# One visit to the attention per tile, with its three parts of TensorE work in a row, in a fused attention and two-MLP kernel

## The reference

```python
for t in range(S):
    kt, vt, rt = k[:, :, t], v[:, :, t], r[:, :, t]
    cur = einsum('bhd,bhe->bhde', u * kt, vt)
    y[:, :, t] = einsum('bhd,bhde->bhe', rt, state + cur)
    state = w * state + einsum('bhd,bhe->bhde', kt, vt)
x = y as (B*S, H*D)
h = x @ w_in1;  x = relu(h)**2 @ w_out1
h = x @ w_in2;  x = (h - tanh(h)) @ w_out2
```

## Time and profile before

| | |
|---|---|
| median of 3 runs | 920.28 us (920.14 to 921.25) |
| the profiled execution | 922.49 us |
| its span in the profile | 920.7 us |
| TensorE matmuls | 896.6 us busy (97% of the span) |
| VectorE / ScalarE / GpSimd | 591.2 / 453.1 / 477.1 us busy |
| TensorE's share of the chain that ended last | 82% |

### The profile page before, as it was taken

One profiled execution on the slowest core, in us unless ns is written; L12 is line 12 of the kernel. 1 busy time (PEld: TensorE's weight loads), 2 busy tenths in 40 slices (PEclk: granted clock), 3 DMA queues, 4 the chain that ended last, 5 costly groups with the idle time before them and its releaser, 6 DMA issues.

```text
span 920.7 us, 13868 instructions
## 1 busy us (share of the span) xinstructions
PE 896.6 (97%) x5340; PEld 736.9 (80%) x5340; DVE 591.2 (64%) x789; ACT 453.1 (49%) x852; POOL 477.1 (52%) x370
## 2 busy tenths in 40 slices
PE   5789999999999999999999999999999999999997
PEld 5668788888888888888888878888888888888886
DVE  6358736545563555445346668778787787787775
ACT  3333414222231322323124477777777777777774
POOL 5543434525443442433225776666666666666664
PEclk9799999999999999999999999999999999999999
DMA  6253111120311112020212200000000000000000
GB/s 254 107 206 140 53 54 54 58 103 1 106 54 54 53 54 106 1 92 16 103 35 69 68 1 1 35 1 1 34 1 1 35 1 0 36 1 1 35 0 35
DMA packets 12162, 47.49 MB, mean 52 GB/s; under 512 B 1472, under 2 KB 1600, under 8 KB 12096
## 3 DMA queue, kind: packets, MB, share of 16 engines
q1 hardware_dynamic: 12096, 46.60, 13.8%
HBM read 41.88 MB, written 4.72 MB: 51 GB/s over the span
## 4 chain that ended last, share of the span: by engine, by line
PE 82%; DVE 8%; POOL 4%; ACT 3%; issue 2%; DMA 1%; ACTq 0%; DVEq 0%; POOLq 0%
PE acc L551 13%; PE acc L553 12%; PE acc L552 12%; PE hid L551 9%; PE hid L552 9%; PE hid L553 9%; PE sc L552 3%; PE sc L553 3%; PE sc L551 3%; PE sc L569 2%; PE y L597 2%; PE sc L605 2%; PE y L583 2%; POOL area L340 1%; DVE area L847 1%
## 5 line engine op out<-in xcount | busy, mean ns | idle before, releaser
L329 POOL TENSOR_TENSOR g_l<-g_f,g_h 128x512 fp32r<-128x512 f32 x96 | 131.6, 1372 | 278.1 <-ACT g_h L413 278.1
L551 PE MATMUL acc<-g_h,wout_h 128*128 128x512 f32 x567 | 225.8, 398 | 0.6 <-POOL g_l L345 0.5
L553 PE MATMUL acc<-g_h,wout_l 128*128 128x512 f32 x567 | 221.9, 391 | 0.0
L552 PE MATMUL acc<-g_l,wout_h 128*128 128x512 f32 x567 | 221.4, 391 | 0.0
L413 ACT ACTIVATE g_h<-g_f 128x512 fp32r<-128x512 f32 x96 | 60.7, 632 | 315.8 <-DVE g_f L790 299.4
L340 POOL TENSOR_TENSOR area<-area 128x512 f32<-128x512 f32 x96 | 125.8, 1311 | 104.6 <-ACT area L431 104.6
L788 DVE TENSOR_SCALAR g_f<-hid 128x512 f32<-128x512 f32 x96 | 66.2, 690 | 164.4 <-PE hid L553 161.5
L551 PE MATMUL hid<-x_h,win_h 128*128 128x512 f32 x432 | 168.5, 390 | 1.2 <-DVE g_f L788 1.2
L552 PE MATMUL hid<-x_l,win_h 128*128 128x512 f32 x432 | 168.1, 389 | 0.0
L553 PE MATMUL hid<-x_h,win_l 128*128 128x512 f32 x432 | 168.0, 389 | 0.0
L345 POOL TENSOR_TENSOR g_l<-g_f,g_h 128x512 fp32r<-128x512 f32 x96 | 128.4, 1338 | 33.6 <-ACT g_h L446 33.6
(11 more groups left out here) (110 smaller groups left out, 1169.7 us busy)
## 6 DMA issues: line engine op xcount, KB each, us to landing
x2T<-in_nat SPq DMA_DIRECT2D x13, 672.0 KB, 5.8
area<-in_nat SPq DMA_DIRECT2D x11, 672.0 KB, 4.9
x2T<-in_tt SPq DMA_DIRECT2D x12, 512.0 KB, 3.8
area<-in_tt SPq DMA_DIRECT2D x11, 512.0 KB, 3.6
out<-x2T SPq DMA_DIRECT2D x18, 256.0 KB, 2.2
x2T<-in_win SPq DMA_DIRECT2D x4, 768.0 KB, 7.7
x2T<-in_wout SPq DMA_DIRECT2D x4, 768.0 KB, 5.0
area<-in_win SPq DMA_DIRECT2D x4, 768.0 KB, 4.4
```

Source lines behind the costliest of these rows:

```text
L329: pool.tensor_tensor(g_l[:, m % 4, :], g_f[:, m % 2, :], g_h[:, m % 4, :].bitcast(F32), ALU.subtract).then_inc(s_gl1, 1)
L551: pe.matmul(dst, wh, xh, start=first, stop=False)
L552: pe.matmul(dst, wh, xl, start=False, stop=False)
L553: return pe.matmul(dst, wl, xh, start=False, stop=last)
```

## The change

The k-v product leaves `attend` and becomes `key_value`: 16 matmuls in tiles of 32 columns with 48 moving columns, which write only the two blocks that are kept (the state's tiles are zeroed once by GpSimd). All of a tile's TensorE work is laid into one place, `slot_at`: steps n = 1, 4, 7, 10, where the score of the *next* tile, then `attend` and `key_value` of this tile follow each other. Since both `score(T+1)` and `key_value(T)` write `sc56`, `key_value(T)` waits for `mask(T+1)`. The mask is placed ahead of `act1` in that step. The products, decay and bonus of a tile move to the step ahead of its score. The transposed part of a tile is loaded after `attend` of tile T-2, the natural part after `key_value`. v is laid out by heads, and rows of w_in need no reordering. At the very end `first2` of the last step is issued one step earlier, and `second2_low_last` serves the last four steps.

```diff
-        def scores_at(i, n):
-            return TPB * (i + 1) + n // 3 if i < BLOCKS - 1 and n < 12 and n % 3 == 0 else None
-        def y_at(i, n):
-            return scores_at(i, n - 1)
-        def x_low_at(i, n):
-            return scores_at(i, n - 2)
+        def slot_at(i, n):
+            return TPB * (i + 1) + n // 3 if 0 <= i < BLOCKS - 1 and n % 3 == 1 and 0 <= n < 12 else None
+        def update_at(i, n):
+            return slot_at(i, n - 1)
+        def decay_k_at(i, n):
+            return slot_at(i, n + 1)
         def prepare_at(i, n):
-            if n == FT - 1:
-                return scores_at(i + 1, 0)
-            return scores_at(i, n + 1)
-        def products_at(i, n):
-            if n >= FT - 2:
-                return scores_at(i + 1, 0) if n == FT - 2 else None
-            return scores_at(i, n + 2)
+            T = slot_at(i, n - 2)
+            if i == 0 and n == 0:
+                return TPB + 1
+            return T + 2 if T is not None and T + 2 < TILES else None
...
             def load_tile(T):
                 before = T - 2 if T > 5 else T - 4
+                sp.wait_ge(s_y, before + 1)
+                load_tt(T)
                 if before < LAST_KV:
                     sp.wait_ge(s_kv, before + 1)
-                else:
-                    sp.wait_ge(s_y, before + 1)
-                load_tt(T)
                 load_nat(T)
...
@@ GpSimd @@
-                    T = prepare_at(i, n)
+                    T = decay_k_at(i, n)
                     if T is not None:
                         decay_k(T)
-                    if i == 0 and n == 0:
-                        decay_k(TPB)
-                    T = products_at(i, n)
+                    T = prepare_at(i, n)
                     if T is not None:
                         products(T)
                     if m + LAG < STEPS:
                         lo1(m + LAG)
...
@@ TensorE @@
-                if T < LAST_KV:
-                    pe.wait_ge(s_kd, T + 1)
-                    for a in range(PAIRS):
-                        mm = pe.matmul(sc_ps(T)[:, VW * a:VW * a + VW], k_of(T)[:, P * a:P * a + P], v[:, a, :],
-                                       start=True, stop=True)
-                    mm.then_inc(s_kv, 1)
+            def key_value(T):
+                if T >= LAST_KV:
+                    return
+                if T >= TPB:
+                    pe.wait_ge(s_scm, T + 2)
+                pe.wait_ge(s_kd, T + 1)
+                for a in range(PAIRS):
+                    for quad in range(4):
+                        at = HP * (quad // 2)
+                        mm = pe.matmul(sc_ps(T)[32 * quad:32 * quad + 32, D * a:D * a + D],
+                                       k_of(T)[:, P * a + 32 * quad:P * a + 32 * quad + 32],
+                                       v_of(T)[:, a, at:at + D], start=True, stop=True)
+                mm.then_inc(s_kv, 1)
...
-                    if scores_at(i, n) is not None:
-                        score(scores_at(i, n))
-                    if y_at(i, n) is not None:
-                        attend(y_at(i, n))
+                    T = slot_at(i, n)
+                    if m == 0:
+                        score(TPB)
+                    if T is not None:
+                        if T + 1 < TILES:
+                            score(T + 1)
+                        attend(T)
+                        key_value(T)
                     second1(m)
             for m in range(STEPS):
-                if m + LAG < STEPS:
+                if m + LAG < STEPS - 1:
                     first2(m + LAG)
+                    if m + LAG == STEPS - 2:
+                        first2(STEPS - 1)
+                if m + LAG < STEPS - 1:
                     second2(m)
                 else:
                     second2_low_last(m)
...
@@ VectorE @@
-                    T = x_low_at(i, n)
+                    T = update_at(i, n)
+                    if T is not None:
+                        update_state(T)
+                    T = slot_at(i, n)
+                    if T is not None and T + 1 < TILES:
+                        mask(T + 1)
+                    if m + LAG < STEPS:
+                        act1(m + LAG)
+                    if m == 0:
+                        mask(TPB)
                     if T is not None:
                         x_low(T)
-                        update_state(T)
-                    if m + LAG < STEPS:
-                        act1(m + LAG)
-                    T = scores_at(i, n)
-                    if T is not None:
-                        mask(T)
                     T = prepare_at(i, n)
                     if T is not None:
                         decay(T)
                         bonus(T)
```

More of the change, by code:

```diff
@@ L91, in build @@
         ident = own.take(P)
-        state = [own.take(PAIRS * 2 * D).rearrange("p (a e) -> p a e", a=PAIRS) for _ in range(B)]
+        state_all = own.take(B * PAIRS * 2 * D)
+        state = [x.rearrange("p (a e) -> p a e", a=PAIRS) for x in
+                 (state_all[:, b * PAIRS * 2 * D:(b + 1) * PAIRS * 2 * D] for b in range(B))]
         scores = [own.take(H * P).rearrange("p (g a t) -> p g a t", g=2, a=PAIRS) for _ in range(2)]
@@ L813, in _ @@
             decay(0)
-            for side, at, width in ((0, 0, 32), (1, 32, 32), (0, 64, 16), (1, 80, 16)):
+            for side, at, width in ((0, 0, D), (1, D, D)):
                 rows = slice(HP * side, HP * side + D)
```

59 lines of the change are left out of this document (26 added, 33 removed).

## The result

The changed kernel takes 932.82 us (median of 4 runs, 931.71 to 932.86) against 920.76 (920.14 to 921.43) beside it: ratio 1.0128 [1.011, 1.0145], slower. The forecast was slower, 942 us, with a range of 922 to 958 that holds the time. The profiled execution has a span of 931.0 us, against 920.7.

What follows compares the result with a forecast made beforehand. TensorE, busy 97% of the span, was taken as the bound. Waits of 26.4 us plus 7 for the clock less gains of 11.8 gave +21.6 on 920.28: 942 us; 931 to 951 (60%), 922 to 958 (8 in 10).

Steps and rivals of the forecast that it cites:

- The nine waits: Blocks 1 to 3, slots n = 4, 7, 10: TensorE's k-v product waits 1.68 us each for the mask, 15.1 us lost.
- rival 1: GpSimd's products not in the way, mask nearly in time: 12 waits of 0.34 us, 912.6 us (910 to 918); 10%.
- Gain 1: One TensorE visit per tile in place of two saves an entry and exit: 0.19 us, 3.6 us for 19 tiles.
- Rival 4: Switching from the score's 64-row tiles directly to 32-column tiles costs 0.2 us, so the joined-visit saving is gone (+3.8).
- Gain 2: Narrow k-v product takes 0.60 us in place of 0.91: 0.31 for 16 tiles, 5.0 us, from -1.3 to +8.6.
- Gains 3 and 4: Ahead of the steps, cheaper k-v products save 2.3 us; at the end, idle ahead of TensorE's last step goes, 0.9.
- The clock: TensorE's granted clock drops behind some of the new waits: five drops, 7 us; none to twelve (17 us) possible.
- Block 0: Late preparation beside weight splits: 0.5 us lost for tile 5, then 3.6 three times, 11.3 us; 5.5 to 15.
- Rival (2): Gains larger, waits small: k-v product at 0.37, block 0 at 5.5, no clock drop: 923.5 us (918 to 931); 15%.

Runs made afterwards that it cites:

- Experiment 8: Changed kernel with GpSimd's products of tiles 5 to 23 on one column only, their diagonals left out of the result: 917.49 us in one run.
- Experiment 4: Changed kernel with GpSimd's products ahead of the scaling of k and VectorE's decay one step earlier: 917.95 us, ratio 0.996 to the kernel before.
- Experiment 3: Changed kernel with GpSimd's products ahead of the scaling of k in the same step: 933.1 us, ratio 1.0121 to the kernel before.
- experiment 10: Changed kernel with VectorE's decay one step earlier, GpSimd's order as in the change: 927.84 us, ratio 1.0067 to the kernel before.
- experiment 1: Changed kernel with the order of work of the kernel before; narrow k-v product, zeroed states and new end stay: 911.56 us, ratio 0.9888.
- experiment 7: Changed kernel with the k-v product as 4 full-array matmuls of 112 moving columns again: 940.79 us, ratio 1.0213 to the kernel before.
- Experiment 6: Kernel before with the new end alone (last first2 a step earlier, four steps of second2_low_last): 920.64 us, ratio 0.9992.
- Experiment 12: Changed kernel with tile 6 loaded ahead of weight unit 7, the last: 932.34 us, ratio 1.012 to the kernel before.
- Experiment 11: Changed kernel with the mask behind act1 again in the slot's step: 930.49 us, ratio 1.0096 to the kernel before.
- experiment 9: Changed kernel, block 0 in old order, then products first and decay a step earlier; block 1's first tile pair prepared over block 0's last four steps: 908.53 us, ratio 0.9864.

## Why the prediction was right, and where its terms were off

The sum was +21.6 us; +10.3 of span were measured. Sign, mechanism and place were right; most of the difference lies in two terms, the k-v product (3.8 us) and the clock (4.3). Every term errs to the same side, towards a slower kernel, so nothing in it is right by errors that cancel; the time lies at the lower end of the main range, 931 to 951.

**The nine waits: right.** Forecast 9 x 1.68 = 15.1, measured 9 x 1.60 = 14.4, in the slots named and in no other of these blocks, the chain within 0.2 us at each step (table above). Experiment 8 shows both parts: 0.39 us from the chain without the products, 1.2 from the turns. Experiment 4 shows that the waits are all that is wrong in blocks 1 to 3. One sentence of it was wrong in its reason: rival 1 said that it decides where the products end. Experiment 3 ended them 1.3 us earlier and changed nothing, for the decay came last; where they end counts only once the decay has moved (experiment 10). In the changed order and in experiment 3 alike two GpSimd ops get a turn before the decay is through.

**Gain 1: right, a little small.** 0.19 us per tile was forecast, from the first matmuls of an entry and an exit. Counted up to the 18th full-width matmul behind a visit, and less the pitch of these, before's score costs 1.32 us and its attend in block 4 1.90 (from 417.64 and 423.04 on TensorE's timeline), the joined visit 2.98 (from 404.32): 0.24 saved, since the pitch is a few ns longer for some matmuls behind an exit too. Block 4, which has no k-v product, agrees: it is 2.06 shorter, 1.32 for the score of tile 20, which moved to block 3, and the rest for three joined visits. With the narrow product in both (experiment 1) it is 0.22. Rival 4 (a price for going from 64-row to 32-column tiles) is excluded: from the score to the attend 1.09 pass in one visit (154.08 to 155.17), and 1.10 from the score to `second` in two (239.86 to 240.96).

**Gain 2: too small.** Forecast 0.31 for each of 16 tiles, 5.0 us; experiment 1 measured 0.55, 8.8 us. From its start to the next `second` the product now takes 0.45 (144.36 to 144.81), and the y part ahead of it, now followed by tiles of its own kind, 0.87 in place of 0.99. So the 0.99 from which I scaled holds 0.12 of exit, which does not shrink with the columns. What does shrink can be read from the starts in experiment 1: with 128 columns groups of four records start 0.109 us apart (the first at 143.49, the eighth at 144.25), with 48 columns 0.042 apart (144.36, 144.66). By columns it would be 0.041. I had placed the product half way towards a pace set by the number of instructions; next to nothing of that is seen. The rule of the Trainium skill (TensorEngine Tiling (Array Packing), Instruction Overhead), counted in columns as I did, would give 0.051 and is too high here. That was my use of it. The overhead that the Trainium skill gives there is about 60 cycles for a matmul. A group's four start within 0.02 us of each other, and the 0.042 us from group to group are some 100 cycles at 2.4 GHz; taken for each of the four, the overhead is below that, and the trace does not speak against it. My 0.46 by the rule met the 0.45 by luck, with the exit in the one and not in the other. Where TensorE waits for the mask the y part's 0.12 goes into the wait, and the product's 0.43 is left (0.91 - 0.48, experiment 7, 1.73 for the four tiles of a block).

**Gains 3 and 4: a little small.** 3.0 for 2.3 ahead of the steps, which experiment 7 gives to the product, and 1.2 for 0.9 behind block 4. Experiment 6 has 1.1 of it in its profile; its runs cannot size it.

**The clock: too dear.** I took five drops, 7 us. There was none at nine waits of 1.4 us in blocks 1 to 3, and two in block 0, at 3.62 and 3.16. By the windows above, these took 5.1 us of full clock (4 us each at 0.57, 0.80, 0.50 and 0.85), some 0.7 of it while TensorE waited, which leaves 4.4 as an estimate. And before's own drop, behind 1.91, did not come again behind 1.77; that had cost 1.7 (1.4 from 60 to 65 us, 0.3 in the 5 us ahead, at 0.94). So the clock costs 2.7 net. I had placed the new waits nearest to the 1.91 of the earlier trace rows. Experiment 1 has the same 1.90 in block 0 (88.88) without a drop, so the length of one idle time isn't by itself what counts.

**Block 0: the size about right, the cause not.** Without its gains (four k-v products and four joined visits, 3.1) and with one score more than before (1.3), block 0 lost 13.0 us with its clock, where 11.3 were forecast without it. Idle time is 9.7 of it and the clock 2.7; the rest is near the 0.18 that the idle times leave out at each of three products (1.42 for 1.60 above). The 0.5 for the product of tile 4 came out as 1.5. The 3.6 for that of tile 5 was right in size and put down to tile 6's load. Experiment 12 excludes that: without a wait for the load 3.4 of 3.6 stay. What is late is lo1, and behind it GpSimd and VectorE in turns, after an act1 that stood behind a split of weights (experiment 12, rows). I also had 3.6 at each of the next two products. That of tile 6 waited 1.5, and the last wait, of 3.16, fell on the score of tile 8, for its decay. Experiment 11, with almost the same waits and no drop, agrees with this split between waits and clock: 1.2 + 4.4, where block 0 is 5.1 shorter.

Rival (2) had the k-v product at 0.37, block 0 at 5.5 and no drop of the clock. Its product came true, and its clock in blocks 1 to 3; block 0 did not, with 9.7 us of idle time and two drops, and so the time lies between it and my figure.

## What to carry to other kernels

Joining three pieces of work on the bound engine saves an entry and an exit (some 0.24 us a tile), and it ties their inputs' deadlines together: a wait of 1.6 us at three tiles of four ate five times that in blocks 1 to 3. Before a deadline is moved a step forward, list the ops with SBUF inputs on VectorE and GpSimd in that step: they go one by one, each engine getting its turn, and what matters is which op is last in line on the way to the deadline, so move that op a step earlier, not its neighbour. And take a change of several parts apart: here the narrow k-v product with the new end makes the kernel 1.1% faster, the order with the old product makes it 2.1% slower, and the order pays a little only after its waits are gone (experiment 9, 1.4% in all).

## What of the hardware was not expected

- Matmuls of 48 columns in 32-column tiles start 0.042 us apart per group of four, those of 128 columns 0.109 (experiment 1), almost exactly as their columns. The exit to full-array matmuls costs some 0.12 beside that (0.99 for 0.87).
- VectorE and GpSimd went strictly in turns wherever both had work waiting in the slots shown: in experiment 3 four ops of the two engines follow each other by turns, and which of GpSimd's ops stands first makes no difference.
- TensorE's granted clock stayed at 2.4 GHz over idle times of 1.42, every 17 us, 1.51, 1.77, 1.90 (experiment 1) and 2.92 (experiment 11). It fell to 1.2 GHz at 3.16, 3.38 and 3.62, but also behind 1.91 and 1.72 (experiment 12), early in the steps. So between 1.7 and 2.9 us both are seen, with 1.72 and 1.77 at the same place of two kernels whose order is the same up to there. What sets the difference stays open.
